# The output product of a three-stage block, computed token-major with 512-wide weights moving

## What is computed

```
x  = attention(q, k, v)            # (8, 576, 512)
x  = moe(x)                        # (8, 576, 512)
h  = max(x @ w_in2, 0)             # (8, 576, 1024)
c  = conv over the tokens, 3 taps, one set of taps per channel
y  = (h * sigmoid(c)) @ w_out2     # (8, 576, 512)
```

## Time and profile before

| | |
|---|---|
| median of 3 runs | 963.47 us (963.39 to 965.4) |
| the profiled execution's own time | 964.72 us |
| its span in the trace | 962.9 us |
| TensorE busy (matmuls) | 932.1 us, 97% |
| VectorE, ScalarE, GpSimd busy | 606.4, 375.1, 345.1 us |
| 128x288 matmuls of the split products (L425) | 5568 |
| 128x512 matmuls of the split products (L417) | 384 |
| mean granted TensorE clock | 0.991 of full speed |

### The profile page before, as it was taken

How to read it: one execution, slowest core, us unless ns; L and a number is a source line. 1 busy time by engine, 2 the same in 40 slices (tenths; PEclk the granted TensorE clock), 3 DMA queues, 4 the chain that set the end, 5 groups by cost and what they waited for, 6 DMA issues and landing times.

```text
span 962.9 us, 16002 instructions
## 1 busy us (share of the span) xinstructions
PE 932.1 (97%) x6652; PEld 906.5 (94%) x6652; DVE 606.4 (63%) x935; ACT 375.1 (39%) x560; POOL 345.1 (36%) x222
## 2 busy tenths in 40 slices
PE   5789999999999999999999999999999999999998
PEld 5589899999998999999989999999999999999998
DVE  6794665657746656576355797775656676756560
ACT  3462443434424434344234254433334343434331
POOL 4742644446426443464204133322222222222220
PEclk8899999999999999999999999999999999999999
DMA  9806116024061160330412302020202010200001
GB/s 309 271 20 187 66 37 199 36 94 164 12 187 65 42 197 34 98 108 12 132 63 81 109 13 75 13 74 26 74 26 75 25 63 25 75 26 26 25 25 50
DMA packets 49911, 77.92 MB, mean 81 GB/s; under 512 B 4272, under 2 KB 22704, under 8 KB 48944
## 3 DMA queue, kind: packets, MB, share of 16 engines
q1 hardware_dynamic: 45232, 67.48, 22.1%
q10 hardware_dynamic: 4608, 9.44, 2.6%
HBM read 56.97 MB, written 18.89 MB: 79 GB/s over the span
## 4 chain that ended last, share of the span: by engine, by line
PE 86%; DVE 8%; issue 2%; DMA 2%; ACT 1%; POOL 1%; ACTq 0%; SPq 0%; DVEq 0%
PE psum L425 71%; PE psum L417 7%; PE psum L483 3%; PE psum L564 2%; PE psum L459 2%; DVE psum L1203 1%; PE psum L518 1%; DMA plain_arena<-in_q 1%; DVE plain_arena L1206 1%; DVE plain_arena L1248 1%; DVE split_arena L1230 1%; DVE plain_arena L1246 1%; POOL plain_arena L1413 0%; DVE split_arena L1366 0%; DMA plain_arena<-in_k 0%
## 5 line engine op out<-in xcount | busy, mean ns | idle before, releaser
L425 PE MATMUL psum<-split_arena 128*128 128x288 f32 x5568 | 762.3, 297 | 15.1 <-DVE plain_arena L1206 5.1
L425 PEld LDWEIGHTS psum<-split_arena 128*128 128x128 f32 x5568 | 749.0, 189 | 20.5 <-DVE plain_arena L1206 7.0
L1492 POOL TENSOR_TENSOR plain_arena<-plain_arena 128x576 f32<-128x576 f32 x64 | 107.5, 1679 | 289.7 <-ACT plain_arena L869 289.7
L1246 DVE TENSOR_SCALAR plain_arena<-plain_arena 128x576 f32<-128x576 f32 x64 | 38.9, 608 | 111.1 <-ACT plain_arena L863 111.1
L1251 DVE SCALAR_TENSOR_TENSOR plain_arena<-plain_arena 128x576 f32<-128x576 f32 x64 | 96.2, 1504 | 2.3
L417 PE MATMUL psum<-split_arena 128*128 128x512 f32 x384 | 95.1, 397 | 0.4 <-DVE split_arena L1128 0.3
L1449 POOL TENSOR_TENSOR plain_arena<-plain_arena 128x576 f32<-128x576 f32 x32 | 46.5, 1454 | 122.4 <-DVE plain_arena L1186 122.4
L417 PEld LDWEIGHTS psum<-split_arena 128*128 128x128 f32 x384 | 71.3, 191 | 15.0 <-DVE split_arena L1128 1.2
L863 ACT ACTIVATE plain_arena<-psum 128x576 f32<-128x576 f32 x64 | 41.4, 649 | 102.8 <-PE psum L425 60.9
L869 ACT ACTIVATE plain_arena<-plain_arena 128x576 f32<-128x576 f32 x64 | 43.7, 682 | 47.8 <-DVE split_arena L1366 41.9
L1186 DVE SCALAR_TENSOR_TENSOR plain_arena<-psum,plain_arena 128x576 f32<-128x576 f32 x32 | 26.2, 818 | 53.8 <-PE psum L564 53.8
(11 more groups left out here) (79 smaller groups left out, 772.9 us busy)
## 6 DMA issues: line engine op xcount, KB each, us to landing
x_dram<-plain_arena ACTq DMA_DIRECT2D x32, 288.0 KB, 2.1
plain_arena<-x_dram SPq DMA_DIRECT2D x8, 1152.0 KB, 5.7
outT<-plain_arena SPq DMA_DIRECT2D x32, 288.0 KB, 2.1
plain_arena<-in_v SPq DMA_DIRECT2D x32, 256.0 KB, 3.3
plain_arena<-in_kT SPq DMA_DIRECT2D x7, 1152.0 KB, 9.5
plain_arena<-in_k SPq DMA_DIRECT2D x7, 1024.0 KB, 5.7
plain_arena<-in_q SPq DMA_DIRECT2D x7, 1024.0 KB, 5.9
plain_arena<-in_w_in SPq DMA_DIRECT2D x8, 512.0 KB, 5.5
```

The lines of the kernel that those rows point to most:

```text
L425: mm = e.matmul(out[:, h, 0:NH], stat[s], mov[m][:, h * NH:(h + 1) * NH], start=first and n == 0, stop=last and n == 2, skip_group_check=True)
L1246: e.tensor_scalar(out, h[:, 1:T + 1], conv[:, f, 1:2], None, ALU.mult).then_inc(conv_chain, 1)
L1492: e.tensor_tensor(gt[:, f % 2, :], gt[:, f % 2, :], hp[:, f % 2, 1:T + 1], ALU.mult).then_inc(hg_full, 1)
```

## The change

The output product is turned round. A tile of hg (128 channels by 128 tokens) is the stationary operand, and a channel tile of `w_out2`, 512 output channels wide, is the moving one. The result has tokens on the partitions and all 512 output channels in one bank. Two batches have 1152 tokens, nine tiles of 128, so the y work goes by pairs of batches: `y_tile(k, t)`, tile t of pair k, has eight f by three matmuls of 512 columns (`three`, which the first block used already). Tile 4 takes 64 tokens of each batch. hg is laid out so that the two batches of a pair stand side by side for each f. Four single banks (4 to 7) take the place of the two pairs. The matmuls of the h units, all work on VectorE and GpSimd, and everything ahead of the last stage stay as they are.

Tiles 0 to 3 of a pair need the even batch alone and run between the h units of the odd one; tiles 4 to 8 run between the h units of the next even batch, with one h unit ahead of tile 4 and two or one behind each of tiles 4 to 7. Tiles 4 to 8 of the last pair stand at the end. Tiles 0 and 4 wait for `hg_lo`, f by f. ScalarE copies 36 tiles of 512 columns in place of 32 of 576, and 36 stores of 256 KB, each one piece of DRAM, replace 32 of 288 KB.

```diff
-        hg = [halves(20992, F2T, T),
-              [grid(split_arena[:, at:at + F2T * T], (F2T, T)) for at in (30208, 0)]]
+        def hg_at(h, f):
+            if h == 0:
+                return 20992 + f * 2 * T
+            return (30208 if f < F2T // 2 else 0) + f % (F2T // 2) * 2 * T
+
+        def hg(h, par, f):
+            at = hg_at(h, f) + par * T
+            return split_arena[:, at:at + T]
+
+        def hg_rows(h, f, t):
+            at = hg_at(h, f) + t * P
+            return split_arena[:, at:at + P]
...
-        yo = plain(X1_AT, 2, T)
+        yo = plain(X1_AT, 2, D)
+        YT = 2 * T // P
+        assert YT == 9 and 2 * T % P == 0
...
-        y_sets = [psum[:, 4:6, :], psum[:, 6:8, :]]
+        y_banks = [psum[:, 4 + i, :] for i in range(4)]
...
+            def store_y(k, ts):
+                for t in ts:
+                    i = k * YT + t
+                    e.wait_ge(y_copied, i + 1)
+                    e.dma_start(out_rows[i * P:(i + 1) * P, :], yo[:, i % 2, :]).then_inc(y_out[i % 2], 16)
 
             load_x2(1)
-
-            def step(b, last=False):
-                if not last:
-                    load_x2(b + 2)
-                store_y(b)
-
-            for i in range(0, B - 2):
-                step(i)
-            step(B - 2, True)
-            step(B - 1, True)
-            for s in y_out:
-                e.wait_ge(s, 32 * B)
+            for b in range(1, B):
+                if b < B - 1:
+                    load_x2(b + 1)
+                store_y((b - 1) // 2, range(4) if b % 2 else range(4, YT))
+            store_y(B // 2 - 1, range(4, YT))
...
-            def y_part(b, par, d, fs):
+            def y_part(k, t, fs):
+                i = k * YT + t
                 if fs[0] == 0:
-                    if b == 0 and d == 0:
+                    if i < 2:
                         e.wait_ge(o_add, B * DT - 1)
-                    elif b == 0 and d == 1:
+                    elif i < 4:
                         e.wait_ge(o_add, B * DT)
                     else:
-                        e.wait_ge(y_copied, b * DT + d - 1)
+                        e.wait_ge(y_copied, i - 3)
                 for f in fs:
-                    if d == 0:
-                        if b == 0:
-                            e.wait_ge(w2_lo, W2_OUT[f // 2] + 1)
-                        e.wait_ge(hg_lo, b * F2T + f + 1)
-                    mm = both_halves(y_sets[d % 2], [w2out[h][:, f, d * P:(d + 1) * P] for h in (0, 1)],
-                                     [hg[par][h][:, f, :] for h in (0, 1)], f == 0, f == F2T - 1)
+                    if t in (0, 4):
+                        e.wait_ge(hg_lo, (2 * k + t // 4) * F2T + f + 1)
+                    if i == 0:
+                        e.wait_ge(w2_lo, W2_OUT[f // 2] + 1)
+                    mm = three(y_banks[i % 4], [hg_rows(h, f, t) for h in (0, 1)],
+                               [w2out[h][:, f, :] for h in (0, 1)], f == 0, f == F2T - 1)
                 if fs[-1] == F2T - 1:
                     mm.then_inc(y_done, 1)
...
+            def odd_batch(b):
+                for t in range(4):
+                    h_unit(b, 2 * t)
+                    h_unit(b, 2 * t + 1)
+                    y_tile(b // 2, t)
+
+            def even_batch(b):
+                h_unit(b, 0)
+                for t in range(4, YT):
+                    y_tile(b // 2 - 1, t)
+                    for f in range(2 * t - 7, min(2 * t - 5, F2T)):
+                        h_unit(b, f)
+
+            for b in range(2, B):
+                if b % 2:
+                    odd_batch(b)
+                else:
+                    even_batch(b)
+            for t in range(4, YT):
+                y_tile(B // 2 - 1, t)
...
-                if f == 0 and not (isinstance(b, int) and b < 2):
-                    e.wait_ge(y_done, (b - 1) * DT)
-                e.activation(hg[par][0][:, f, :], gt[:, f % 2, :], ACT.Identity).then_inc(hg_hi, 1)
+                if f == 0 and b >= 2:
+                    e.wait_ge(y_done, b // 2 * YT if b % 2 else (b // 2 - 1) * YT + 5)
+                e.activation(hg(0, par, f), gt[:, f % 2, :], ACT.Identity).then_inc(hg_hi, 1)
...
-            def copy_y(b, d):
-                e.wait_ge(y_done, b * DT + d + 1)
-                if d >= 2:
-                    e.wait_ge(y_out[d % 2], b * 32 + 16)
-                elif isinstance(b, int) and b == 0:
-                    e.wait_ge(x1_out[d], 32 * B)
+            def copy_y(k, t):
+                i = k * YT + t
+                e.wait_ge(y_done, i + 1)
+                if i >= 2:
+                    e.wait_ge(y_out[i % 2], i // 2 * 16)
                 else:
-                    e.wait_ge(y_out[d % 2], b * 32)
-                e.activation(yo[:, d % 2, :].rearrange("p (a b) -> p a b", a=2), y_sets[d % 2][:, :, 0:NH],
-                             ACT.Identity).then_inc(y_copied, 1)
-
-            def step(b, par, last=False, x=True):
-
-                for d in range(DT):
-                    if not last:
-                        tile_steps(b + 1, 1 - par, 2 * d)
-                        if d == DT - 1 and x:
-                            hi_x2(b + 2)
-                        tile_steps(b + 1, 1 - par, 2 * d + 1)
-                        if d == DT - 1:
-                            tile_steps(b + 1, 1 - par, F2T)
-                            tile_steps(b + 1, 1 - par, F2T + 1)
-                    copy_y(b, d)
+                    for x in x1_out:
+                        e.wait_ge(x, 32 * B)
+                e.activation(yo[:, i % 2, :], y_banks[i % 4], ACT.Identity).then_inc(y_copied, 1)
+
+            def last_tiles(b):
+                if b < B - 1:
+                    hi_x2(b + 1)
+                for f in range(F2T - 1, F2T + 2):
+                    tile_steps(b, b % 2, f)
+
+            def odd_batch(b):
+                for t in range(4):
+                    tile_steps(b, 1, 2 * t)
+                    if t < 3:
+                        tile_steps(b, 1, 2 * t + 1)
+                    else:
+                        last_tiles(b)
+                    copy_y(b // 2, t)
+
+            def even_batch(b):
+                tile_steps(b, 0, 0)
+                for t in range(4, YT):
+                    copy_y(b // 2 - 1, t)
+                    for f in range(2 * t - 7, min(2 * t - 5, F2T - 1)):
+                        tile_steps(b, 0, f)
+                    if t == YT - 2:
+                        last_tiles(b)
```

More of the change, by code:

```diff
@@ L26, with build @@
 BANK = 512
-def build(nc, q, kT, k, v, w_in, g_ln, w_sgT, b_sg, w_out, w_in2, conv_w, w_out2, outT):
+def build(nc, q, kT, k, v, w_in, g_ln, w_sgT, b_sg, w_out, w_in2, conv_w, w_out2, out_rows):
     B, T, D = q.shape
@@ L390, in _ @@
                 e.dma_start(staged(stage_w2[n % 3], hi), src).then_inc(w2_raw[n % 3], 16)
[L392 to L409 removed]
+            def store_y(k, ts):
[3 more added lines that the diff above has]
+                    e.dma_start(out_rows[i * P:(i + 1) * P, :], yo[:, i % 2, :]).then_inc(y_out[i % 2], 16)
+            load_x2(1)
+            for b in range(1, B):
[3 more added lines that the diff above has]
+            store_y(B // 2 - 1, range(4, YT))
+            for n, s in enumerate(y_out):
+                e.wait_ge(s, 16 * (B // 2 * YT // 2))
         @block.tensor
@@ L676, in _, with y_tile @@
             body(B - 1, None)
-            def y_part(b, par, d, fs):
+            def y_part(k, t, fs):
+                i = k * YT + t
                 if fs[0] == 0:
-                    if b == 0 and d == 0:
+                    if i < 2:
                         e.wait_ge(o_add, B * DT - 1)
-                    elif b == 0 and d == 1:
+                    elif i < 4:
                         e.wait_ge(o_add, B * DT)
                     else:
-                        e.wait_ge(y_copied, b * DT + d - 1)
+                        e.wait_ge(y_copied, i - 3)
                 for f in fs:
-                    if d == 0:
-                        if b == 0:
-                            e.wait_ge(w2_lo, W2_OUT[f // 2] + 1)
-                        e.wait_ge(hg_lo, b * F2T + f + 1)
-                    mm = both_halves(y_sets[d % 2], [w2out[h][:, f, d * P:(d + 1) * P] for h in (0, 1)],
-                                     [hg[par][h][:, f, :] for h in (0, 1)], f == 0, f == F2T - 1)
+                    if t in (0, 4):
[4 more added lines that the diff above has]
+                               [w2out[h][:, f, :] for h in (0, 1)], f == 0, f == F2T - 1)
                 if fs[-1] == F2T - 1:
                     mm.then_inc(y_done, 1)
[L697 to L702, removed]
-                    if not last:
-                        h_unit(b + 1, 2 * d)
-                        h_unit(b + 1, 2 * d + 1)
-                    y_unit(b, par, d)
+            def y_tile(k, t):
+                y_part(k, t, list(range(F2T)))
             def first_y(f):
-                y_part(0, 0, 0, [f])
-                y_part(0, 0, 1, [f])
+                y_part(0, 0, [f])
```

(28 more changed lines are left out.)

4 lines of the change are left out of this document (1 added, 3 removed).

## The result

| | before | changed |
|---|---|---|
| median of 6 runs | 963.98 us (963.39 to 965.4) | 957.31 us (955.77 to 959.09) |
| profiled execution, its own time | 964.72 us | 955.77 us |
| its span | 962.9 us | 953.9 us |

The ratio is 0.9931, with a 95% interval from 0.991 to 0.9952: faster by 6.7 us, where 6.3 was forecast.

A forecast was written before the change was run, and what follows sets the result against it. TensorE's matmuls were taken to bound the kernel from 583.44 us on. Removing 196.9 us, adding 190.65 and saving 0.06 on the last copy gave -6.3 us: 958.4 profiled, 957.2 median, range 955.0 to 960.2.

The forecast's parts named there:

- The bound: From 583.44 us to the end, only the number of TensorE matmuls and the distance between their starts count.
- The mechanism: Last stage: most loss beyond columns at 2.4 GHz goes with the instruction; 864 wide matmuls replace 1536 narrow ones.
- What the two widths cost: Matmul times from the trace before: 133.4 ns for 288 columns, 228.6 for 512, 13.4 and 15.3 above their columns.
- 834 x 228.6 ns = 190.65: Time in us added to the long piece by wide matmuls, against 196.9 us removed: net -6.25 us.
- The start: First pieces of tiles 0 and 1: 1.15 us saved, but absorbed as the wait for hg tile 5 grows to about 3.
- h unit 0 of batch 1: Behind the start's wait, its last quarter is due just as `lo_x2` ends: cost 0 to 0.2 us, taken as 0.
- Tile 4: Needs all odd-batch hg tiles sooner than before; slack 0.4, 1.8, 1.8, 1.4 us at batches 1, 3, 5, 7, no wait.
- Columns alone govern: Rival: last-stage wide matmuls take 237.1 ns, 5.69 us a tile, about 964.3 us in all; chance 0.07.
- The tile 4 rival: The odd batch's hg chain comes later and tile 4 waits; at 4 us later 4.3 us slower, 967.8; chance 0.04.
- The four more copies and stores: Cost nothing: TensorE needs a bank back some 25 us later, and ScalarE has over 200 us idle.

The follow-up runs named there:

- one product less: The changed kernel with the product of high hg and low weights left out of every y tile, 16 matmuls for 24: 905.89 us, 51.5 below the change.
- tile 4 first: The changed kernel with h unit 0 of the even batches moved behind tile 4: 964.35 us, ratio 1.0011 to the kernel before.
- other banks: The changed kernel with the last four tiles worked two and two in turn, each matmul writing another bank than the one ahead: 957.42 us.

## Why the prediction was right

- **The bound.** TensorE alone sets the end from 583.44 us on: it did before and does after. In the run with one product less, 63 us of its matmuls went, the long piece became 49.8 us shorter, and the 7 us of waits that came back stand at tile 4, but for 0.4.
- **The mechanism**, a cost per matmul beside its columns: shown by the run at 256 columns, and the layout, the banks and the turned operands shown to be worth nothing.
- **The size of it** was off. The step is "What the two widths cost": 228.6 ns for a wide matmul, a mean over two short stretches. By 226.7 and 133.3 ns those stretches would take 7.04 and 4.53 us, and they took 7.07 and 4.59, the second right behind four transposes; what the 0.03 and 0.06 us are is not settled. In the last stage there is no such surplus: a tile and two h units take 5.46 + 6.38 = 11.84 us, which is 24 x 226.7 + 48 x 133.3. And 133.3, 120.0 and 226.7 ns all are columns / 2.4 plus 13.3: the fixed cost is the same at every width, and does not grow from 13.4 to 15.3. With 133.3 and 226.7 the term "834 x 228.6 ns = 190.65" is 189.1, and the net of the long piece -7.7 for the forecast -6.25; the trace has -7.2, and 0.26 of the difference is the next item.
- **The start.** The 1.15 us of TensorE time saved ahead of 583.44 were mostly absorbed by the wait, 2.7 us in two parts for "about 3" in one, and the gain from filling it shows that work fits into it for nothing. What the prediction did not have is that the longer wait can bring the clock down: 1.3 us in some executions, none in the two traces of the change.
- **h unit 0 of batch 1**, taken as 0 with a bound of 0.2: 3.44 to 3.45 us where 3.18 is the rule, so it cost 0.26, just outside; the wait is for the low part of x, as forecast.
- **Tile 4.** Reserves forecast 0.4, 1.8, 1.8 and 1.4 us. In the changed trace batch 1's last h unit ends at 617.47 and the last low part at 627.93 + 2.41 = 630.34, while tile 4 asks for it at 626.12 + 21 x 0.2267 = 630.9: 0.5 us, for 0.4. The experiment that took 3.2 us away found waits of 2.2 and 1.3, which is 3.2 less 1.0 and less 1.9. At batch 1 the last low part came 11.95 us after the last h unit there (620.99 to 632.94), not 12.87: without h unit 0 behind tile 3 the hg chain itself was 0.9 us earlier.
- **The rivals.** "Columns alone govern" would have shown 5.69 us a tile; it is 5.46. The Trainium skill's 2.5 ns a matmul ("TensorE: Matmul & The Clock Gate", "Wait — 56ns, not 53.3ns?") does not hold for these float32r matmuls; 13.3 does, at three widths. The tile 4 rival named a real mechanism, as the run with tile 4 first shows, but the hg chain was not the 3.4 us later that it needed.
- **The four more copies and stores** cost nothing visible: a copy takes 594 ns, a store lands in 2.0 us. (At the very end TensorE needs a bank back after three tiles, 16.4 us, not "some 25"; that is room enough for a copy.)

That the median came out within 0.2 us of the forecast is partly luck: the long piece gave 0.9 us more than forecast, the median of before rose by 0.5 us from three runs to six, and on the chips of the experiments it lay up to 1.1 us higher still.

## What to carry to other kernels

Where TensorE is the bound and its matmuls run back to back, count instructions as well as columns: the widest moving operand the bank allows is worth 13.3 ns for each matmul it does away with, 4.4% of the cost of a column between 288 and 512 columns here, and a matmul so short that the next stationary tile's load no longer fits under it (111 ns) costs far more. A regrouped product also needs its inputs at other moments. Work out for each when they are needed and when they are there, from the trace of before, and keep one unit of other work in front of the one with the least reserve. Count a wait of a few us on TensorE at more than its length, since the clock may drop behind it.

## What was not expected of the hardware

- What is taken here for the load of 128 stationary columns, 111 ns, hides under the one matmul ahead of it and no more: 384 + 128 columns took 284.6 ns where 256 + 256 took 240.0, for the same columns and count.
- The fixed 13.3 ns is the same to a tenth at 256, 288 and 512 columns, in one bank or in turn, and with equal or new stationary tiles. What it is stays open.
- Waits close together had a second price. In the run with one product less the granted clock fell to 0.50 of full behind waits of 2.15 and 2.44 us and again, to 0.56 to 0.59, behind one of 1.67, 4.5 us in all, where the waits themselves were some 12. With the change's own waits at the start of the stage it fell in three traces (256 columns, other banks, tile 4 first) and not in the two of the change, for 1.3 us each time that it could be read. What decides between the two stays open.
